# Layer-2 transposes in two row tiles of 64 tokens, with the output matmuls behind both halves

## The chip, the cores and the metric

The kernel runs on one core of one Trainium2 chip. The metric is the device time in microseconds (us) of one execution; three executions of the kernel before were timed, and their median counts. One further execution was recorded by the hardware profiler.

## What is computed

Banded attention with sinks (2 batches x 8 heads x 768 tokens, head size 64) gives 1536 token rows of 512. A first feed-forward layer (512 to 2048 to 512, squared ReLU) and a second one follow. The change is in the second layer:

```python
def _moe2_ref(x, w_in, w_out, g_ln):        # x: 1536 x 512, w_in: 512 x 1024, w_out: 1024 x 512
    h = x @ w_in
    e = np.exp(h - np.max(h, axis=-1, keepdims=True))
    sm = e / (np.sum(e, axis=-1, keepdims=True) + 1e-09)
    solu = h * sm
    mu, var = mean(solu), mean((solu - mu) ** 2)     # over the 1024 features of a token
    ln = (solu - mu) / np.sqrt(var + 1e-06) * g_ln
    return ln @ w_out
```

## The kernel before, in words

The program is written per engine, by hand: each engine runs its own list of instructions in order, and semaphores with counts tie the lists together. Nothing is scheduled by a planner. float32 matrices are split into a high and a low part (type fp32r), and each product is three matmuls: high x high, high x low, low x high.

The second layer works on 12 tiles of 128 tokens (`TILES2`). For tile i TensorE runs four pieces:

- `expand` (L1052): the tile's input, transposed, times `w_in`: 24 matmuls of 128 x 512 into two PSUM banks.
- ScalarE and VectorE then make the normed tile: VectorE the negated maximum (L849), ScalarE the exponential (L597), VectorE the product (L853), the statistics (L859 to L866), ScalarE the square root (L609), VectorE the normed rows (L874, semaphore `normed_ready`). In between VectorE also does `ln_low` of the tile before (L839) and `y_low` of a later one (L814).
- `turn_normed` (L1059): eight transposes of 128 tokens x 128 features, written as matmuls against an identity. The first four fill bank `LT_BANK`, the last four the next bank; each group of four tells `ln_turned`.
- ScalarE copies each bank to `ln_hi` (`ln_high`, L592), VectorE makes `ln_lo` from bank and `ln_hi` (`ln_low`, L839, semaphore `ln_lo_done`).
- `contract` (L1073): `ln` transposed times `w_out`, 12 matmuls for chunks 0 to 3 (half 0) and 12 for chunks 4 to 7 (half 1), into an output bank that ScalarE copies out (L587).

TensorE interleaves three tiles. In `steps(k)`, for tile i: `expand(i)`, `contract(i-2)` half 0, `turn_normed(i-1)`, `contract(i-2)` half 1. Ahead of the loop stand `expand(0)`, `expand(1)` and `turn_normed(0)`; behind it `contract(10)` half 0, `turn_normed(11)`, `contract(10)` half 1 and both halves of `contract(11)`. The first of these steps are written out, the middle ones are a hardware loop, whose waits compare with register values.

The attention part has transposes of another form: `turn` (L915) turns 64 rows x 128 columns at a time, rows 0 to 63 into one bank and rows 64 to 127 into the next, one behind the other. Trace rows name the shape of the array used: `128*128` for all rows and columns, `64*128` for half the rows, `128*64` for half the columns.

Of the kernel before, what the change touches and what calls it, by code (L numbers as in the profile page):

```python
# [8 lines left out]
P = 128  # L9
# [20 lines left out]
FC2 = D_FF2 // P  # L30
TILES2 = TOKENS // P
# [8 lines left out]
def build(nc, q_t, k_t, v, limits_in_dram, w1_in, w1_out, w2_in, w2_out, g_ln, out):  # L40
    F32, F32R, I32, U32 = mybir.dt.float32, mybir.dt.float32r, mybir.dt.int32, mybir.dt.uint32
    ALU, ACT, AX = mybir.AluOpType, mybir.ActivationFunctionType, mybir.AxisListType
# [26 lines left out]
    identity = keep.take("identity", [P, P])  # L69
# [77 lines left out]
    normed = mlp2.take("normed", [P, 2, D_FF2])  # L147
    assert mlp2.at <= BASE + 32 * KIB
    ln_hi = mlp2.take("ln_hi", [P, 2, FC2, P], F32R)
    ln_lo = mlp2.take("ln_lo", [P, 2, FC2, P], F32R)  # L150
# [14 lines left out]
    ps = nc.alloc_psum_tensor("ps", [P, 8, 512], F32)  # L165
    S_BANK, PT_BANK, X_BANK = 0, 4, 6
    H_BANK, Y_BANK = 0, 4
    LT_BANK, O_BANK = 4, 6
# [22 lines left out]
    HQ = P // 2  # L191
# [12 lines left out]
    def sem(name):  # L204
        return nc.alloc_semaphore(name)
# [67 lines left out]
    normed_ready = sem("normed_ready")  # L273
    ln_turned = sem("ln_turned")
    ln_hi_done = sem("ln_hi_done")
    ln_lo_done = sem("ln_lo_done")
# [4 lines left out]
    def wait(eng, semaphore, count):  # L281

        if isinstance(count, int) and count <= 0:
            return
        eng.wait_ge(semaphore, count)
# [14 lines left out]
    with block as block:  # L300
# [170 lines left out]
        def _(act):  # L471
# [115 lines left out]
                nc.scalar.activation(out_sb[:, u, :], ps[:, O_BANK + u, :], ACT.Copy).then_inc(out_ready, 1)  # L587

            def ln_high(i, u):
                for half in range(2):  # L590
                    act.wait_ge(ln_turned, 2 * i + half + 1)
                    nc.scalar.activation(ln_hi[:, u, 4 * half:4 * half + 4, :].rearrange("p a b -> p (a b)"), ps[:, LT_BANK + half, :], ACT.Copy).then_inc(ln_hi_done, 1)  # L592

            def tile(k, u, first, last):
                i = 2 * k + u
                act.wait_ge(ff_max_done, i + 1)
                nc.scalar.activation(expo[:, u, :], ps[:, f_bank(u):f_bank(u) + HALF2, :].rearrange("p a b -> p (a b)"),  # L597
                                     ACT.Exp, bias=ff_negmax[:, u:u + 1], accum_out=ff_sum[:, u:u + 1]).then_inc(ff_exp_done, 1)
                if first and u == 0:
                    y_out(TILES1 - 1)  # L600
                if first and u == 1:
                    act.wait_ge(y_out_dve, 2 * TILES1)
                    act.wait_ge(y_out_act, 2 * TILES1)
                if not (first and u == 0):
                    ln_high(i - 1, 1 - u)
                if not last:
                    y_high(i + 2, u)
                act.wait_ge(var_ready, i + 1)
                nc.scalar.activation(std[:, u:u + 1], var_b[:, u:u + 1], ACT.Sqrt).then_inc(std_ready, 1)  # L609
                if not first:  # L610
                    out_copy(k - 1, i - 2, u)
# [6 lines left out]
            for u in range(2):  # L618
                tile(TILES2 // 2 - 1, u, False, True)
            ln_high(TILES2 - 1, 1)  # L620
            for u in range(2):
                out_copy(TILES2 // 2 - 1, TILES2 - 2 + u, u)

        @block.vector
        def _(dve):
# [208 lines left out]


            def ln_low(i, u):
                for half in range(2):
                    dve.wait_ge(ln_hi_done, 2 * i + half + 1)
                    dve.tensor_tensor(ln_lo[:, u, 4 * half:4 * half + 4, :].rearrange("p a b -> p (a b)"), ps[:, LT_BANK + half, :],  # L839
                                      ln_hi[:, u, 4 * half:4 * half + 4, :].rearrange("p a b -> p (a b)"), ALU.subtract).then_inc(ln_lo_done, 1)  # L840

            STATS = 6

            def tile(k, u, first, last):
# [10 lines left out]
                if not (first and u == 0):  # L855
                    ln_low(i - 1, 1 - u)
# [25 lines left out]
            for u in range(2):  # L882
                tile(TILES2 // 2 - 1, u, False, True)
            ln_low(TILES2 - 1, 1)

        @block.tensor
        def _(pe):
# [158 lines left out]
            def expand(i, u):  # L1046

                pe.wait_ge(y_ready, i + 1)
                for f in range(HALF2):
                    for c in range(DC):  # L1050
                        for m, (y, w) in enumerate(((y_hi, w2_in_hi), (y_hi, w2_in_lo), (y_lo, w2_in_hi))):
                            last = mm(ps[:, f_bank(u) + f, :], y[:, u, c, :], w[:, c, 512 * f:512 * (f + 1)],  # L1052
                                      start=(c == 0 and m == 0), stop=(c == DC - 1 and m == 2))
                last.then_inc(ff_done, 1)

            def turn_normed(i, u):
                pe.wait_ge(normed_ready, i + 1)
                for f in range(FC2):
                    last = nc.tensor.transpose(ps[:, LT_BANK + f // 4, (f % 4) * P:(f % 4 + 1) * P],  # L1059
                                               normed[:, u, f * P:(f + 1) * P], identity[:, :])  # L1060
                    if f % 4 == 3:
                        last.then_inc(ln_turned, 1)

            def contract(i, u, half):

                pe.wait_ge(ln_lo_done, 2 * i + half + 1)
                if half == 0:
                    wait(pe, out_ready, i - 1)
                    if isinstance(i, int) and i < 2:
                        pe.wait_ge(y_out_dve, 2 * TILES1)  # L1070
                for f in range(FC2 // 2 * half, FC2 // 2 * (half + 1)):
                    for m, (a, w) in enumerate(((ln_hi, w2_out_hi), (ln_hi, w2_out_lo), (ln_lo, w2_out_hi))):
                        last = mm(ps[:, O_BANK + u, :], a[:, u, f, :], w[:, f, :], start=(f == 0 and m == 0), stop=(f == FC2 - 1 and m == 2))  # L1073
                if half == 1:
                    last.then_inc(out_done, 1)
# [35 lines left out]
                project(t, FC1 - 1, 1, False, True)  # L1111
            expand(1, 1)
            pe.wait_ge(y_out_act, 2 * TILES1)
            turn_normed(0, 0)

            def steps(k):
                for u in range(2):
                    i = 2 * k + u
                    expand(i, u)
                    contract(i - 2, u, 0)  # L1120
                    turn_normed(i - 1, 1 - u)
                    contract(i - 2, u, 1)

            steps(1)
            with pe.Fori(2, TILES2 // 2) as k:
                steps(k)
            contract(TILES2 - 2, 0, 0)
            turn_normed(TILES2 - 1, 1)
            contract(TILES2 - 2, 0, 1)
            for half in range(2):  # L1130
# [39 lines left out]
```

## Time and profile before

| | before |
|---|---|
| median of 3 runs | 498.95 us (497.9 to 500.12) |
| the profiled execution, its own time | 499.36 us |
| its span in the profile | 497.6 us |
| TensorE busy | 481.1 us (97%) |
| VectorE, ScalarE, GpSimd busy | 287.4, 248.0, 106.7 us |
| granted TensorE clock, whole span | 1.0 of full speed |
| second layer's stretch on TensorE | from about 350 us to the end |

The span runs from the first to the last instruction of the program; the 1.8 us between it and the execution's own time lie around it. TensorE is busy nearly throughout; a time that the second layer loses or gains on TensorE is seen one to one in the end time, as long as nothing else is late.

### The profile page before, as it was taken

What the parts mean: (1) busy time and instruction counts of PE and PEld (TensorE: products, weight loads), DVE (VectorE), ACT (ScalarE), POOL (GpSimd) and SP (SyncE); (2) the same over time, 40 slices, a digit from 0 to 9 for tenths busy, and PEclk for the clock granted to TensorE, in tenths of its full rate; (3) what the DMA queues carried; (4) which work ended last, traced back from release to release, by engine and by line L of the source; (5) the groups of instructions that cost most, each with busy time, mean ns of one, the idle gap of its engine ahead of it and who ended that gap; (6) DMA issues with size and microseconds to landing.
All of it is one profiled execution on the core that took longest, in us unless ns stands there. A gap on an engine that the chain in (4) does not pass through costs nothing.

```text
span 497.6 us, 7811 instructions
## 1 busy us (share of the span) xinstructions
PE 481.1 (97%) x2742; PEld 387.4 (78%) x2742; DVE 287.4 (58%) x678; ACT 248.0 (50%) x539; POOL 106.7 (21%) x129
## 2 busy tenths in 40 slices
PE   6889897999999999999999999999999999999997
PEld 3656575787888888888888888888888888888885
DVE  5788776368677454334435433444497666666651
ACT  3978878433443453344345334434356555545441
POOL 1876666049998000000000000000000000000000
PEclk9999999999999999999999999999999999999999
DMA  6768821170000000000000000000000000000001
GB/s 199 290 238 308 316 98 36 44 297 0 0 0 0 0 1 1 0 0 0 0 1 0 0 1 0 0 0 1 0 1 22 22 21 21 21 21 21 21 28 57
DMA packets 10138, 25.97 MB, mean 52 GB/s; under 512 B 3200, under 2 KB 5248, under 8 KB 8832
## 3 DMA queue, kind: packets, MB, share of 16 engines
q1 hardware_dynamic: 10112, 25.64, 14.1%
q8 instruction: 14, 0.23, 0.2%
q14 instruction: 12, 0.10, 0.1%
HBM read 22.48 MB, written 3.15 MB: 52 GB/s over the span
## 4 chain that ended last, share of the span: by engine, by line
PE 86%; ACT 6%; DVE 3%; DMA 3%; SPq 1%; POOL 1%; issue 1%; DVEq 0%
PE ps L1023 26%; PE ps L1038 26%; PE ps L1073 13%; PE ps L1052 13%; ACT probs L480 3%; PE ps L1059 2%; DMA k_sb<-in_k_t 2%; PE ps L951 2%; PE ps L906 1%; PE ps L915 1%; PE ps L961 1%; ACT pt_sb L488 1%; SPq L320 1%; POOL probs L402 1%; ACT x_hi L494 1%
## 5 line engine op out<-in xcount | busy, mean ns | idle before, releaser
L790 DVE CAST act_hi<-act_sq 128x512 fp32r<-128x512 f32 x48 | 26.0, 542 | 126.1 <-ACT act_sq L538 123.3
L533 ACT ACTIVATE ps<-ps 128x512 f32<-128x512 f32 x48 | 27.9, 582 | 141.4 <-PE ps L1023 141.4
L1023 PE MATMUL ps<-x_hi,w_in_hi 128*128 128x512 f32 x192 | 75.1, 391 | 0.0
L1038 PE MATMUL ps<-act_hi,w_out_hi 128*128 128x512 f32 x192 | 74.8, 390 | 0.1
L1023 PE MATMUL ps<-x_hi,w_in_lo 128*128 128x512 f32 x192 | 74.8, 389 | 0.0
L1023 PE MATMUL ps<-x_lo,w_in_hi 128*128 128x512 f32 x192 | 74.7, 389 | 0.0
L1038 PE MATMUL ps<-act_hi,w_out_lo 128*128 128x512 f32 x192 | 74.7, 389 | 0.0
L1038 PE MATMUL ps<-act_lo,w_out_hi 128*128 128x512 f32 x192 | 74.7, 389 | 0.0
L402 POOL TENSOR_TENSOR probs<-probs,row_inv 128x512 f32<-128x512 f32 (+1 forms) x48 | 45.7, 973 | 30.8 <-DVE row_inv L691 30.8
L480 ACT ACTIVATE probs<-probs,neg_max 128x272 f32<-128x272 f32 (+2 forms) x96 | 46.7, 497 | 7.1 <-DVE neg_max L678 7.0
L1023 PEld LDWEIGHTS ps<-x_hi,w_in_hi 128*128 128x128 f32 x192 | 36.0, 188 | 8.5 <-issue 1.2
L1038 PEld LDWEIGHTS ps<-act_hi,w_out_hi 128*128 128x128 f32 x192 | 36.1, 188 | 8.0 <-DVE w_out_lo L795 0.6
L1023 PEld LDWEIGHTS ps<-x_lo,w_in_hi 128*128 128x128 f32 x192 | 36.1, 188 | 7.6
L1038 PEld LDWEIGHTS ps<-act_lo,w_out_hi 128*128 128x128 f32 x192 | 36.0, 188 | 7.5
L1038 PEld LDWEIGHTS ps<-act_hi,w_out_lo 128*128 128x128 f32 x192 | 36.0, 188 | 7.4
L1023 PEld LDWEIGHTS ps<-x_hi,w_in_lo 128*128 128x128 f32 x192 | 36.0, 188 | 7.4
L1073 PE MATMUL ps<-w_out_hi,ln_hi 128*128 128x512 f32 x96 | 38.4, 400 | 0.0
L795 DVE TENSOR_TENSOR w_out_lo<-w_out_raw,w_out_hi 128x512 fp32r<-128x512 f32 x48 | 38.3, 798 | 0.0
L792 DVE TENSOR_TENSOR act_lo<-act_sq,act_hi 128x512 fp32r<-128x512 f32 x48 | 37.0, 771 | 1.7
L1073 PE MATMUL ps<-w_out_hi,ln_lo 128*128 128x512 f32 x96 | 37.5, 391 | 0.0
L1052 PE MATMUL ps<-w_in_hi,y_hi 128*128 128x512 f32 x96 | 37.4, 390 | 0.0
L1052 PE MATMUL ps<-w_in_hi,y_lo 128*128 128x512 f32 x96 | 37.4, 389 | 0.0
(97 smaller groups left out, 829.3 us busy)
## 6 DMA issues: line engine op xcount, KB each, us to landing
w_in_raw<-in_w_in SPq DMA_DIRECT2D x4, 1024.0 KB, 4.8
w_out_raw<-in_w_out SPq DMA_DIRECT2D x4, 1024.0 KB, 8.2
k_sb<-in_k_t SPq DMA_DIRECT2D x8, 408.0 KB, 5.1
q_sb<-in_q_t SPq DMA_DIRECT2D x8, 384.0 KB, 4.2
v_sb<-in_v SPq DMA_DIRECT2D x16, 192.0 KB, 3.9
out<-out_sb SPq DMA_DIRECT2D x12, 256.0 KB, 2.0
w_in_raw<-in_w_in SPq DMA_DIRECT2D x1, 2048.0 KB, 9.4
w_out_raw<-in_w_out SPq DMA_DIRECT2D x1, 2048.0 KB, 13.8
```

The source lines that it names most:

```text
L402: return pool.tensor_tensor(rows, rows, inv.to_broadcast(list(rows.shape)), ALU.mult)
L480: last = nc.scalar.activation(probs[:, b, u, cols], probs[:, b, u, cols], ACT.Exp, scale=-1.0, bias=neg_max[:, b, u, i:i + 1], accum_out=r ...
L533: nc.scalar.activation(ps[:, H_BANK + u, :], ps[:, H_BANK + u, :], ACT.Relu).then_inc(relu_done, 1)
L790: dve.tensor_copy(act_hi[:, u, :], act_sq[:, u, :]).then_inc(act_hi_done, 1)
L792: dve.tensor_tensor(act_lo[:, u, :], act_sq[:, u, :], act_hi[:, u, :], ALU.subtract).then_inc(act_lo_done, 1)
L795: dve.tensor_tensor(w1_out_lo[:, u, :], src, w1_out_hi[:, u, :], ALU.subtract).then_inc(w1_out_ready, 1)
L951: mm(ps[HEAD_DIM * u:HEAD_DIM * (u + 1), X_BANK + col // HALF, col % HALF:col % HALF + size], v_sb[:, b, u, j, :], pt_sb[:, j, width * u + ...
L1023: last = mm(ps[:, H_BANK + u, :], w[:, u, c, :], x[:, c, t * TILE1:(t + 1) * TILE1], start=(c == 0 and m == 0), stop=(c == DC - 1 and m == 2))
L1038: last = mm(ps[:, Y_BANK + c, :], w[:, u, c * P:(c + 1) * P], a[:, u, :], start=(first and m == 0), stop=(final and m == 2), skip_group_ch ...
L1052: last = mm(ps[:, f_bank(u) + f, :], y[:, u, c, :], w[:, c, 512 * f:512 * (f + 1)], start=(c == 0 and m == 0), stop=(c == DC - 1 and m == 2))
L1059: last = nc.tensor.transpose(ps[:, LT_BANK + f // 4, (f % 4) * P:(f % 4 + 1) * P], normed[:, u, f * P:(f + 1) * P], identity[:, :])
L1073: last = mm(ps[:, O_BANK + u, :], a[:, u, f, :], w[:, f, :], start=(f == 0 and m == 0), stop=(f == FC2 - 1 and m == 2))
```

## The change

The eight transposes of 128 x 128 become sixteen of 64 tokens x 128 features: for every chunk first tokens 0 to 63 (rows 0 to 63 of the array) into bank `LT_BANK`, then tokens 64 to 127 into the next bank. A bank now holds one half of the tokens of all eight chunks, and its semaphore is told at the last chunk. `ln_high` and `ln_low` read one bank each as before, and write 64 of every 128 columns. `contract` half 0 needs all tokens, so it waits for both parts of `ln_lo`; the wait in half 1 falls away. The wait for `normed_ready` moves out of `turn_normed` to the matmuls of chunk 3 in `contract` (three matmuls ahead of the transposes), and for tile 0 ahead of the first call.

```diff
             def ln_high(i, u):
-                for half in range(2):
-                    act.wait_ge(ln_turned, 2 * i + half + 1)
-                    nc.scalar.activation(ln_hi[:, u, 4 * half:4 * half + 4, :].rearrange("p a b -> p (a b)"), ps[:, LT_BANK + half, :], ACT.Copy).then_inc(ln_hi_done, 1)
+                for h in range(2):
+                    act.wait_ge(ln_turned, 2 * i + h + 1)
+                    turned_half = ps[:, LT_BANK + h, :].rearrange("p (f q) -> p f q", q=HQ)
+                    nc.scalar.activation(ln_hi[:, u, :, HQ * h:HQ * (h + 1)], turned_half, ACT.Copy).then_inc(ln_hi_done, 1)
...
             def turn_normed(i, u):
-                pe.wait_ge(normed_ready, i + 1)
+
                 for f in range(FC2):
-                    last = nc.tensor.transpose(ps[:, LT_BANK + f // 4, (f % 4) * P:(f % 4 + 1) * P],
-                                               normed[:, u, f * P:(f + 1) * P], identity[:, :])
-                    if f % 4 == 3:
-                        last.then_inc(ln_turned, 1)
+                    for h in range(2):
+                        half = slice(HQ * h, HQ * (h + 1))
+                        last = nc.tensor.transpose(ps[:, LT_BANK + h, f * HQ:(f + 1) * HQ], normed[half, u, f * P:(f + 1) * P], identity[half, half])
+                        if f == FC2 - 1:
+                            last.then_inc(ln_turned, 1)
 
             def contract(i, u, half):
 
-                pe.wait_ge(ln_lo_done, 2 * i + half + 1)
                 if half == 0:
+                    pe.wait_ge(ln_lo_done, 2 * i + 2)
                     wait(pe, out_ready, i - 1)
                     if isinstance(i, int) and i < 2:
                         pe.wait_ge(y_out_dve, 2 * TILES1)
                 for f in range(FC2 // 2 * half, FC2 // 2 * (half + 1)):
+                    if f == FC2 // 2 - 1:
+                        if not (isinstance(i, int) and i == TILES2 - 1):
+                            pe.wait_ge(normed_ready, i + 2)
                     for m, (a, w) in enumerate(((ln_hi, w2_out_hi), (ln_hi, w2_out_lo), (ln_lo, w2_out_hi))):
...
             expand(1, 1)
             pe.wait_ge(y_out_act, 2 * TILES1)
+            pe.wait_ge(normed_ready, 1)
             turn_normed(0, 0)
```

`ln_low` on VectorE changes as `ln_high` does.

TensorE's list at the middle of a loop step, around `turn_normed` (`normed` is what is turned, `ln_hi` and `ln_lo` feed the output matmuls). Before:

```order
L1073 MATMUL ps<-w_out_hi,ln_hi 128x512
L1073 MATMUL ps<-w_out_lo,ln_hi 128x512
L1073 MATMUL ps<-w_out_hi,ln_lo 128x512
L1059 MATMUL ps<-identity,normed 128x128 [waits normed_ready]
L1059 MATMUL ps<-identity,normed 128x128 x7
L1066 REGISTER_ALU
L1073 MATMUL ps<-w_out_hi,ln_hi 128x512 [waits ln_lo_done]
```

The same place with the change:

```order
L1079 MATMUL ps<-w_out_hi,ln_hi 128x512 [waits normed_ready]
L1079 MATMUL ps<-w_out_lo,ln_hi 128x512
L1079 MATMUL ps<-w_out_hi,ln_lo 128x512
L1063 MATMUL ps<-identity,normed 128x64 x16
L1079 MATMUL ps<-w_out_hi,ln_hi 128x512
```

The wait for `normed_ready` has moved three matmuls ahead, eight transposes have become sixteen, and half 1 starts without a wait.

TensorE's list at the start of the last tile's `contract`, behind the last `contract(10)` matmul. Before, where half 1 waits once more twelve matmuls later:

```order
L1073 MATMUL ps<-w_out_hi,ln_lo 128x512
L1073 MATMUL ps<-w_out_hi,ln_hi 128x512 [waits out_ready,ln_lo_done]
L1073 MATMUL ps<-w_out_lo,ln_hi 128x512
L1073 MATMUL ps<-w_out_hi,ln_lo 128x512
...
L1073 MATMUL ps<-w_out_hi,ln_lo 128x512
L1073 MATMUL ps<-w_out_hi,ln_hi 128x512 [waits ln_lo_done]
L1073 MATMUL ps<-w_out_lo,ln_hi 128x512
```

With the change:

```order
L1079 MATMUL ps<-w_out_hi,ln_lo 128x512
L1079 MATMUL ps<-w_out_hi,ln_hi 128x512 [waits out_ready,ln_lo_done]
L1079 MATMUL ps<-w_out_lo,ln_hi 128x512
L1079 MATMUL ps<-w_out_hi,ln_lo 128x512
L1079 MATMUL ps<-w_out_hi,ln_hi 128x512
```

The one wait left stands where half 0's stood, and asks for both parts of `ln_lo`.

## Rows read from the trace of the kernel before

**Rows 1.** The page: busy time by engine, and the granted clock in 40 slices.
```profile
PE 481.1 (97%) x2742; PEld 387.4 (78%) x2742; DVE 287.4 (58%) x678; ACT 248.0 (50%) x539; POOL 106.7 (21%) x129
PEclk9999999999999999999999999999999999999999
```

**Rows 2.** Chain that ended last, second layer: start us, us, what, instructions.
```profile
423.52 5.44 PE ps L1052 x24
428.96 2.72 PE ps L1073 x12
431.69 0.87 PE ps L1059 x8
432.56 2.74 PE ps L1073 x12
```

**Rows 3.** Timeline of TensorE around one turn, 430.9 to 433.2 us.
```profile
431.07 0.39 PE L1073 MATMUL ps<-w_out_lo,ln_hi 128*128 128x512 f32 x1
431.29 0.39 PE L1073 MATMUL ps<-w_out_hi,ln_lo 128*128 128x512 f32 x1
431.53 1.03 PE L1059 MATMUL ps<-identity,normed 128*128 128x128 f32 x8
432.32 0.48 PE L1073 MATMUL ps<-w_out_hi,ln_hi 128*128 128x512 f32 x1
432.63 0.40 PE L1073 MATMUL ps<-w_out_lo,ln_hi 128*128 128x512 f32 x1
```

**Rows 4.** Timeline of TensorE, cut at 88.66, then at 88.76 us.
```profile
88.64 0.28 PE L915 MATMUL ps<-identity,probs 64*128 64x64 f32 x2
...
88.64 0.34 PE L915 MATMUL ps<-identity,probs 64*128 64x64 f32 x4
```

**Rows 5.** Timeline of TensorE at the end of attention, 88.0 to 90.9 us.
```profile
88.32 0.39 PE L1023 MATMUL ps<-x_lo,w_in_hi 128*128 128x512 f32 x1
88.64 0.59 PE L915 MATMUL ps<-identity,probs 64*128 64x64 f32 x12
89.06 0.23 PE L915 MATMUL ps<-identity,sink_probs 64*128 64x64 f32 x2
89.21 1.09 PE L951 MATMUL ps<-pt_sb,v_sb 128*64 128x128 f32 x12
90.23 0.50 PE L1023 MATMUL ps<-x_hi,w_in_hi 128*128 128x512 f32 x1
90.57 0.40 PE L1023 MATMUL ps<-x_hi,w_in_lo 128*128 128x512 f32 x1
```

**Rows 6.** Durations, in ns (min/median/max), of half transposes and half-column matmuls of the attention.
```profile
L915 PE MATMUL ps<-identity,probs x352: 216/223/275, 14.6 to 89.0; 64*128 64x64 f32 x176
...
L951 PE MATMUL ps<-pt_sb,v_sb x12: 272/298/379, 89.2 to 89.9; 128*64 128x128 f32 x8, 128*64 128x256 f32 x4
```

**Rows 7.** Timeline, 371.4 to 372.6 us: TensorE, its weight loads, VectorE.
```profile
371.65 0.39 PE L1073 MATMUL ps<-w_out_hi,ln_lo 128*128 128x512 f32 x1
371.88 0.39 PE L1073 MATMUL ps<-w_out_hi,ln_hi 128*128 128x512 f32 x1
...
372.37 0.33 PEld L1059 LDWEIGHTS ps<-identity,normed 128*128 128x128 f32 x2
...
371.51 0.81 DVE L874 TENSOR_SCALAR normed<-solu,mean_var,row_gain 128x1024 f32<-128x1024 f32 x1
```

**Rows 8.** Timeline of ScalarE and VectorE before the last turn, and of TensorE.
```profile
479.32 1.09 ACT L592 ACTIVATE ln_hi<-ps 128x512 fp32r<-128x512 f32 x2 [0.69 <-PE ps L1059]
...
479.80 0.14 DVE L854 TENSOR_SCALAR ff_den<-ff_sum 128x1 f32<-128x1 f32 x1
479.95 1.29 DVE L839 TENSOR_TENSOR ln_lo<-ps,ln_hi 128x512 fp32r<-128x512 f32 x2
483.85 0.81 DVE L874 TENSOR_SCALAR normed<-solu,mean_var,row_gain 128x1024 f32<-128x1024 f32 x1
486.29 1.29 DVE L839 TENSOR_TENSOR ln_lo<-ps,ln_hi 128x512 fp32r<-128x512 f32 x2 [1.62 <-ACT ln_hi L592]
...
484.33 0.39 PE L1073 MATMUL ps<-w_out_hi,ln_hi 128*128 128x512 f32 x1
```

**Rows 9.** The same chain: the tail, from the last turn to the end.
```profile
485.19 0.87 PE ps L1059 x8
486.06 8.22 PE ps L1073 x36
```

**Rows 10.** Timeline of ScalarE and VectorE in a tile of the loop.
```profile
432.16 1.09 ACT L592 ACTIVATE ln_hi<-ps 128x512 fp32r<-128x512 f32 x2 [0.70 <-PE ps L1059]
...
437.01 0.81 DVE L874 TENSOR_SCALAR normed<-solu,mean_var,row_gain 128x1024 f32<-128x1024 f32 x1
```

More of the change, by code:

```diff
@@ L836, in ln_low @@
             def ln_low(i, u):
[L837 to L840, printed above, removed]
+                for h in range(2):
+                    dve.wait_ge(ln_hi_done, 2 * i + h + 1)
+                    queries = slice(HQ * h, HQ * (h + 1))
+                    turned_half = ps[:, LT_BANK + h, :].rearrange("p (f q) -> p f q", q=HQ)
+                    dve.tensor_tensor(ln_lo[:, u, :, queries], turned_half, ln_hi[:, u, :, queries], ALU.subtract).then_inc(ln_lo_done, 1)
             STATS = 6
@@ L1056, in turn_normed @@
             def turn_normed(i, u):
-                pe.wait_ge(normed_ready, i + 1)
                 for f in range(FC2):
-                    last = nc.tensor.transpose(ps[:, LT_BANK + f // 4, (f % 4) * P:(f % 4 + 1) * P],
-                                               normed[:, u, f * P:(f + 1) * P], identity[:, :])
-                    if f % 4 == 3:
-                        last.then_inc(ln_turned, 1)
+                    for h in range(2):
+                        half = slice(HQ * h, HQ * (h + 1))
+                        last = nc.tensor.transpose(ps[:, LT_BANK + h, f * HQ:(f + 1) * HQ], normed[half, u, f * P:(f + 1) * P], identity[half, half])
+                        if f == FC2 - 1:
+                            last.then_inc(ln_turned, 1)
             def contract(i, u, half):
-                pe.wait_ge(ln_lo_done, 2 * i + half + 1)
                 if half == 0:
+                    pe.wait_ge(ln_lo_done, 2 * i + 2)
                     wait(pe, out_ready, i - 1)
```

## The prediction, before the run

> **What bounds the kernel now.** I read the page first: TensorE is busy 97% of the span at the full granted clock, every other engine 58% or less [rows 1]. So the second layer is worth what it costs on TensorE, unless another engine becomes late. Next the chain that ended last: in the second layer it runs through TensorE alone, in a pattern that repeats every 11.78 us: 24 expanding matmuls, 12 output matmuls, 8 transposes in 0.87 us, 12 output matmuls [rows 2]. There are 12 such turns, 12 x 0.87 = 10.4 us in all, and this is what the change touches. Then the timeline around one turn, read by starts, because ends overlap: from the last full matmul's start at 431.29 to the second full one's start behind the turn at 432.63, 1.34 us go by [rows 3]. That is the measure I compare. In it, the first transpose follows the last matmul by 0.24, the eight take 0.109 each, and the first full matmul behind them holds the next back for 0.31 where 0.227 is usual.
>
> **Part 1: sixteen half transposes for eight whole ones.** The attention has exactly the new form (64*128 array, 64 rows, identity of 64), and once it stands directly behind full 128*128 matmuls, so every step has a row [rows 4 to 6].
>
> - Entry. The last full matmul starts at 88.32, the first pair of halves at 88.64 [rows 5]: 0.32. Before it was 0.24. The array has to run empty before it changes shape; no weights are loaded ahead.
> - The pairs. Two halves start together: a matmul of 0.27 and its partner span 0.28 [rows 4]. A second pair ends 0.34 - 0.28 = 0.06 later; as its matmuls take 0.223 where the first two took 0.27, it starts 0.11 behind the first. From there to the sixth pair the end moves from 0.34 to 0.59 [rows 4, 5], four steps of 0.0625. Eight pairs: 0.11 + 6 x 0.0625 = 0.485 from the first start to the last. Before, 7 x 0.109 = 0.76.
> - Exit. From the last pair at 89.06 to the next shape at 89.21: 0.15 [rows 5]. Before it was 0.03 (last transpose at 432.29, matmul at 432.32 [rows 3]; 432.29 is 431.53 + 1.03 less the 0.27 that one takes).
> - The first full matmul behind an empty array: 90.23 to 90.57, 0.34 [rows 5], against 0.31.
>
> The sum is 0.32 + 0.485 + 0.15 + 0.34 = 1.295 against 1.34: **a turn gains 0.04 us**, 12 turns 0.5 us. The transposes proper get 0.27 shorter, and the two changes of shape take back 0.23. The switch from 64*128 straight back to 128*128 is in no row; I take the one to 128*64, and bound it by 0.03 (as free as today) and by 0.31 (behind the half-column matmuls of 128*64, which end at 89.21 + 1.09 = 90.30 and take 0.379 each, a full one starts at 90.23, 0.31 behind the last start [rows 5, 6]). It should be nearest to the row of its own kind, the half transpose, behind which 23 changes of shape in the attention lie at 0.15 to 0.19, so I stay at 0.15. With the low bound a turn gains 0.16, with the high one it loses 0.12.
>
> A page of the Trainium skill, "TensorEngine Tiling (Array Packing)", section Key Properties, says that a change of tiling mode drains the array. Another, "TensorE: Matmul & The Clock Gate", section Single matmul latency, gives a lone bf16 matmul of N columns (398+N)/2.4 ns, 0.38 us for 512 and 0.19 for 64. An estimate with these as the two drains would make a turn dearer by 0.06 and 0.04 than my sum, so that it loses 0.06 in place of gaining 0.04, and the kernel would take some 1.0 us more; the trace's 0.32 and 0.15 are shorter, and I use them.
>
> **Part 2: the wait for the normed tile, three matmuls earlier.** In the loop it costs nothing: the tile is ready at 437.82 [rows 10] and the turn that uses it comes at about 443.3, one 11.78 us period behind 431.53. Twice there is no such slack.
>
> - Turn of tile 1. VectorE ends the tile at 372.32, and TensorE's weight load for the transposes starts at 372.37, just in time [rows 7]. The wait now sits on the matmul that started at 371.88. It would start at 372.37, 0.49 late, with nothing loaded ahead (0.34 in place of 0.227, so 0.11 more): 0.61 us later than before. The 0.04 that turn 0 gained is swallowed.
> - Turn of tile 11. The tile is ready at 484.66 [rows 8]; the matmul that now waits started at 484.33 [rows 8]. With 0.05 for the signal that is 0.38. A bank is now complete only at the end of the turn: ScalarE started 0.63 behind the first transpose (432.16 against 431.53 [rows 10, 3]); now it is 0.08 (later entry) + 0.485 + 0.22 + 0.04, some 0.2 later. `ln_lo`, which started at 479.95 right behind 479.80 + 0.14 [rows 8], is then held up by 0.15, and the statistics and the normed tile behind it on VectorE too. So 0.53, and 0.11 for the empty array: 0.64. Turn 10's gain is swallowed as well.
>
> Turns 1 to 9 and 11 keep their gain, 10 x 0.04 = 0.4. **Net: 0.61 + 0.64 - 0.4 = +0.85 us.**
>
> **Part 3: output matmuls behind both halves.** In the loop `ln_lo` is done one whole `expand` (5.44) before its use; nothing. Only the end is close: the last `ln_lo` ended at 487.58 [rows 8], and the last tile's matmuls start at 486.06 + 2.74 = 488.80 [rows 9, 2]. The later bank costs 0.25 of that 1.2 us. Nothing again, and without that cover it would come at most to those 0.25 us. `ln_hi` and `ln_lo` are written in pieces of 64 elements; both are off the path, with 5 us of slack in the loop, so this costs nothing unless they double.
>
> **The sum** against the profiled execution's own 499.36 us: 500.2. That execution stands 0.4 above the median of 498.95, so for the median of runs I forecast **499.8 us**.
>
> **The rivals.**
>
> 1. *The earlier wait is harmless* (the halves and loads flow around it, or it holds nothing back). Then only the 12 x 0.04 stay: 498.5. Against it: both tiles are ready later than the matmul that now asks for them [rows 7, 8]. Chance 0.12.
> 2. *Row tiling doubles the rate and the changes of shape are hidden.* A turn falls from 0.87 to 0.435. The two late waits stay, and swallow turns 0 and 10: 0.61 + 0.64 - 10 x 0.435 = -3.1, so 495.8, faster. Against it: pairs come every 0.0625, but the 0.32 and 0.15 around them are in the trace [rows 5]. The Trainium skill, "TensorEngine Tiling (Array Packing)", section Theoretical Speedup, states up to 2x for a dimension of 64 or less; the attention's rows bear this out inside a block (0.0625 for a pair against 0.109), not at its edges. Chance 0.07.
> 3. *The halves do not overlap here*, slower: each takes its own slot of 0.0625, 14 or so in place of 7. A block of 16 then takes 0.11 + 14 x 0.0625 = 0.99 in place of 0.485, 0.5 a turn; 10 turns lose 0.46 each: 0.61 + 0.64 + 4.6 = 5.9, so 504.8. It decides from about 0.02 us between the halves of a pair on. For it: the banks and operands are new. Against it: 352 rows of the attention at 0.22 [rows 6], in pairs [rows 4]. Chance 0.05.
> 4. *The way back to the full shape is dearer*, up to the 0.31 bound: 0.16 a turn more, +1.6, so 501.4, or with more than that slower. Chance 0.08, half of it above the bound of "same".
>
> That the change does not do what it says can hardly be: the list of instructions shows sixteen transposes and the moved wait.
>
> **How the numbers follow.** My own case has 0.68. A measurement of this kernel can tell about 0.5%, 2.5 us, from no change: below 496.45 is faster, above 501.45 slower. Same: 0.68 + 0.12 + 0.04 = 0.84; slower: 0.05 + 0.04 = 0.09; faster: 0.07. The range takes in rival 1 and the bounds of the exit (a gain of 0.16 a turn would give 498.6, a loss of 0.12 some 501.4) and a little for the scatter of a median: 498.0 to 501.6.
>
> **What would show it right or wrong.** In the new trace: halves starting in pairs 0.06 apart; from the last full matmul's start to the second full one's behind the turn about 1.30 us; the period still about 11.74; TensorE idle some 0.5 us at two places only, ahead of the fourth chunk in the first and the last `contract` before a turn, with VectorE's normed tile named as releaser; the last `ln_lo` done about 0.9 us before it is wanted. A distance of 0.95 or less would mean the shape changes are hidden; 1.45 or more would be rival 3 or 4; no idle time at the two places, rival 1.

## The result, and the profile after

| | before | changed |
|---|---|---|
| median of 12 runs | 498.75 us (497.71 to 500.12) | 499.91 us (499.03 to 500.82) |
| ratio to before | | 1.0026, 95% interval 1.0017 to 1.0036 |
| span of the profiled execution | 497.6 us | 499.0 us |
| TensorE, first `expand` matmul to the last matmul's start | 144.00 us | 144.97 us |
| from the last full matmul to the second full one behind a turn (typical) | 1.337 us | 1.299 us |

The change costs 1.2 us (1.16 between the medians; the interval says 0.8 to 1.8). The forecast was 0.85 us over a median of 498.95, so 499.8. The fourth line takes the second layer alone: the stretch ahead of it varies by some 1.5 us between profiled executions, whatever the kernel (the first `expand` started between 348.8 and 350.4 us), while one kernel that was profiled twice (e1 and e9 below) had second layers of 143.574 and 143.573 us. It grew by 0.97 us, which lies inside the interval for the whole kernel. The ratios of the experiments below leave out two slow executions, one of e1 (541.4 us) and one of the kernel before beside it (1230.16 us), which the medians keep.

The page of the changed kernel, busy time by engine, and the granted clock, against [rows 1]:

```profile
PE 482.6 (97%) x2838; PEld 384.6 (77%) x2838; DVE 285.3 (57%) x678; ACT 248.1 (50%) x539; POOL 107.4 (22%) x129
PEclk9999999999999999999999999999999999999999
```

There are 96 matmuls more (8 more for each of 12 turns). The granted clock and the counts of the other engines are as before; VectorE's busy time is 2.1 us less and that of the weight loads 2.8 us less, neither of them the bound. The timeline of TensorE around one turn of the loop, against [rows 3] (start us, us, engine, line, operation, count):

```profile
431.99 0.39 PE L1079 MATMUL ps<-w_out_lo,ln_hi 128*128 128x512 f32 x1
432.22 0.39 PE L1079 MATMUL ps<-w_out_hi,ln_lo 128*128 128x512 f32 x1
432.54 0.71 PE L1063 MATMUL ps<-identity,normed 64*128 64x64 f32 x16
433.18 0.50 PE L1079 MATMUL ps<-w_out_hi,ln_hi 128*128 128x512 f32 x1
433.52 0.40 PE L1079 MATMUL ps<-w_out_lo,ln_hi 128*128 128x512 f32 x1
```

"Full" matmuls are those of 128x512 on the whole array, "halves" the half transposes. Read it by starts: 0.32 to the first half, then 0.49 to the last one (0.71 less the 0.22 that one takes), 0.15 to the first full matmul, 0.34 to the second: 1.30 us. The same view cut at 432.6 and at 432.7 us shows the pairs, as [rows 4] do:

```profile
432.54 0.28 PE L1063 MATMUL ps<-identity,normed 64*128 64x64 f32 x2
...
432.54 0.34 PE L1063 MATMUL ps<-identity,normed 64*128 64x64 f32 x4
```

Two halves end 0.28 us after the start, four 0.34: the partners of a pair start together, within 4 ns, and a second pair costs 0.06. In the 12 turns the distance from the last full matmul to the second one behind the turn is 1.299 to 1.304; before it was 1.332 to 1.339.

What pays for this saving, and more, are two idle times. TensorE ahead of the turns of tile 1 and tile 11, against [rows 7, 8] (in brackets the idle time and its releaser):

```profile
372.08 0.39 PE L1079 MATMUL ps<-w_out_hi,ln_lo 128*128 128x512 f32 x1
372.85 0.50 PE L1079 MATMUL ps<-w_out_hi,ln_hi 128*128 128x512 f32 x1 [0.38 <-DVE normed L876]
373.19 0.39 PE L1079 MATMUL ps<-w_out_lo,ln_hi 128*128 128x512 f32 x1
...
484.87 0.39 PE L1079 MATMUL ps<-w_out_hi,ln_lo 128*128 128x512 f32 x1
485.71 0.50 PE L1079 MATMUL ps<-w_out_hi,ln_hi 128*128 128x512 f32 x1 [0.45 <-DVE normed L876]
```

From start to start 0.77 us and 0.84 us go by where 0.227 is usual: 0.54 and 0.61 us lost. The matmul behind is followed at 0.34 in place of 0.227, so 0.11 more each. No other gap in the second layer's matmuls is longer than a turn's own. VectorE's end of the normed tile fits: 371.99 + 0.81 = 372.80, and 0.05 later the matmul starts; for tile 11 it is 484.84 + 0.81 = 485.65, and 0.06.

```profile
371.99 0.81 DVE L876 TENSOR_SCALAR normed<-solu,mean_var,row_gain 128x1024 f32<-128x1024 f32 x1
...
484.84 0.81 DVE L876 TENSOR_SCALAR normed<-solu,mean_var,row_gain 128x1024 f32<-128x1024 f32 x1
```

The sum for the second layer: 0.54 + 0.61 + 2 x 0.11 - 12 x 0.038 = 0.91 us, of 0.97 measured. The rest, some 0.05, is spread over the 559 ordinary steps from one full matmul to the next, which take 227.35 ns in the mean and took 227.26 before; why is not shown.

The later bank can be seen on VectorE before the turn of tile 11, against [rows 8]:

```profile
480.59 0.14 DVE L856 TENSOR_SCALAR ff_den<-ff_sum 128x1 f32<-128x1 f32 x1
480.95 1.29 DVE L842 TENSOR_TENSOR ln_lo<-ps,ln_hi 128x512 fp32r<-128x512 f32 x2 [0.21 <-ACT ln_hi L593]
```

Before, `ln_lo` started 0.15 behind `ff_den` and did not wait for ScalarE; now it starts 0.36 behind and does: 0.21 later, and all that stands behind it on VectorE with it.

The joint wait ahead of the last tile's output matmuls is met in time. The last `ln_lo` ended at 487.98 + 1.29 = 489.27, and the first matmul that needs it started at 490.12, at the usual distance behind the one ahead of it:

```profile
487.98 1.29 DVE L842 TENSOR_TENSOR ln_lo<-ps,ln_hi 128x512 fp32r<-128x512 f32 x2 [2.33 <-ACT ln_hi L593]
```

### The profile page after: what moved, and what is told of

Its sections match the earlier page's. It is cut to its first block, busy times and chain, and to the rows that moved or that the text cites. A ratio compares the mean times of both kernels' runs of the same rounds, so it can differ in the third digit from the quotient of the medians.

```text
span 499.0 us, 7995 instructions
## 1 busy us (share of the span) xinstructions
PE 482.6 (97%) x2838; PEld 384.6 (77%) x2838; DVE 285.3 (57%) x678; ACT 248.1 (50%) x539; POOL 107.4 (22%) x129
## 4 chain that ended last, share of the span: by engine, by line
PE 84%; ACT 5%; DVE 4%; DMA 2%; SPq 1%; issue 1%; POOL 1%; DVEq 0%
PE ps L1025 26%; PE ps L1040 26%; PE ps L1079 12%; PE ps L1054 12%; ACT probs L480 3%; DMA k_sb<-in_k_t 2%; PE ps L908 2%; PE ps L953 2%; PE ps L1063 1%; PE ps L917 1%; PE ps L963 1%; ACT pt_sb L488 1%; SPq L320 1%; POOL probs L402 1%; ACT x_hi L494 1%
## 5 line engine op out<-in xcount | busy, mean ns | idle before, releaser
L791 DVE CAST act_hi<-act_sq 128x512 fp32r<-128x512 f32 x48 | 21.5, 448 | 128.2 <-ACT act_sq L538 125.3
L793 DVE TENSOR_TENSOR act_lo<-act_sq,act_hi 128x512 fp32r<-128x512 f32 x48 | 38.4, 799 | 1.7
L782 DVE TENSOR_TENSOR w_in_lo<-w_in_raw,w_in_hi 128x512 fp32r<-128x512 f32 x48 | 37.7, 787 | 1.7 <-ACT w_in_hi L523 1.7
L1079 PE MATMUL ps<-w_out_lo,ln_hi 128*128 128x512 f32 x96 | 37.4, 390 | 0.0
```

The costliest lines, as they stand in the source:

```text
L782: dve.tensor_tensor(w1_in_lo[:, u, :, :], src, w1_in_hi[:, u, :, :], ALU.subtract).then_inc(w1_in_ready, 1)
L791: dve.tensor_copy(act_hi[:, u, :], act_sq[:, u, :]).then_inc(act_hi_done, 1)
L793: dve.tensor_tensor(act_lo[:, u, :], act_sq[:, u, :], act_hi[:, u, :], ALU.subtract).then_inc(act_lo_done, 1)
```

## The experiments

The first question was whether the loss comes from the two late waits or from something spread over the turns. Intervals are of the ratio to runs of the kernel before on the same chip. The ratios differ a little from the quotients of the medians beside them (e2: 500.20 / 498.73 = 1.0029), and the intervals hold both. "Second layer" is the fourth line of the table above, read from each profile.

| run | ratio, 95% interval | median, us | before, us | second layer against before |
|---|---|---|---|---|
| e1_wait_at_turn | 0.9987 (0.9972 to 1.0001) | 498.39 | 498.73 | -0.42 |
| e2_wait_alone | 1.0020 (1.0004 to 1.0036) | 500.20 | 498.73 | +1.08 |
| e3_both_halves_alone | 1.0007 (0.9998 to 1.0016) | 499.22 | 498.73 | -0.03 |
| e4_wait_at_chunk_0 | 1.0176 (1.0159 to 1.0194) | 507.47 | 498.73 | +8.22 |
| e5_rows_in_turn | 1.0061 (1.0040 to 1.0082) | 502.21 | 499.15 | +3.21 |
| e6_turn_in_two_parts | 1.0075 (1.0048 to 1.0102) | 502.89 | 499.15 | +4.00 |
| e7_wait_at_chunk_2 | 1.0046 (1.0028 to 1.0063) | 501.17 | 498.78 | +2.31 |
| e8_wait_at_chunk_1 | 1.0096 (1.0077 to 1.0115) | 503.59 | 498.78 | +3.73 |
| e9_wait_at_turn_again | 0.9997 (0.9984 to 1.0010) | 498.65 | 498.78 | -0.43 |

### Row tiles without the two late waits

```diff
             def turn_normed(i, u):
+                if isinstance(i, int):
+                    pe.wait_ge(normed_ready, i + 1)
...
-                    if f == FC2 // 2 - 1:
-                        if not (isinstance(i, int) and i == TILES2 - 1):
-                            pe.wait_ge(normed_ready, i + 2)
+                    if f == FC2 // 2 - 1 and not isinstance(i, int):
+                        pe.wait_ge(normed_ready, i + 2)
...
-            pe.wait_ge(normed_ready, 1)
             turn_normed(0, 0)
```

Only the written-out steps have whole numbers for i, and these hold the turns of tiles 0, 1, 2 and 11.

> The row-tiled transposes stay; at the turns of tiles 1, 2 and 11 (and 0) the wait for the normed tile goes back to the first transpose, in the loop it stays at chunk 3, where the tile is long ready. Theory (two late waits cost 0.61 and 0.64 us, the row-tiled turns gain 0.04 each): 12 x 0.04 = 0.5 us faster than before, some 1.7 us faster than the change's 499.9. TensorE never idle ahead of those turns. Rival (the loss is spread over all turns, in the changes of array shape): no better than the change, about 1.1 us slower than before.

Measured: ratio 0.9987, second layer 0.42 us shorter than before. The timeline of TensorE at the turn of tile 11:

```profile
484.42 0.39 PE L1079 MATMUL ps<-w_out_hi,ln_lo 128*128 128x512 f32 x1
484.73 0.72 PE L1064 MATMUL ps<-identity,normed 64*128 64x64 f32 x16
485.38 0.50 PE L1079 MATMUL ps<-w_out_hi,ln_hi 128*128 128x512 f32 x1
```

The 0.32 to the first half is that of every turn; nothing waits. With the waits where they were, the change's loss of 0.97 turns into a gain of 0.42. The same kernel was run once more, with 11 executions beside the 12 of the first time:

> The first of these experiments once more, for a narrower interval: row-tiled transposes, the wait of tiles 0, 1, 2 and 11 at their first transpose. Theory: 0.4 to 0.5 us faster than before, ratio 0.999. Rival (the gain seen in the trace is given back elsewhere): ratio 1.000 or more.

The second layer gained the same 0.43 us, but the ratio is 0.9997 with 1 inside the interval. So the gain is plain in the trace, and the time of the whole kernel does not resolve it. Against the change the version is clearly better (its intervals end at 1.0001 and 1.0010, that of the change begins at 1.0017); against the kernel before it is no better that one could measure.

### The wait alone

In the kernel before, with its whole transposes, the waits stand as in the change (same lines as in the diff of the change), and nothing else is touched.

> The kernel before with its whole 128x128 transposes, and only the wait for the normed tile moved to chunk 3 of the output matmuls. Theory: tile 1 costs 0.49 + 0.11 = 0.60 us, tile 11 costs 0.38 + 0.11 = 0.49 us (its normed tile is not held up by a later bank): 1.1 us slower than before. Rival (the wait hurts only together with the row tiles): equal to before within 0.2 us.

Measured 1.0020, second layer +1.08 us. TensorE idles at the same two places:

```profile
371.45 0.39 PE L1076 MATMUL ps<-w_out_hi,ln_lo 128*128 128x512 f32 x1
372.17 0.50 PE L1076 MATMUL ps<-w_out_hi,ln_hi 128*128 128x512 f32 x1 [0.33 <-DVE normed L874]
...
484.49 0.39 PE L1076 MATMUL ps<-w_out_hi,ln_lo 128*128 128x512 f32 x1
485.10 0.50 PE L1076 MATMUL ps<-w_out_hi,ln_hi 128*128 128x512 f32 x1 [0.22 <-DVE normed L874]
```

Lost are 713 - 227 = 486 ns and 606 - 227 = 379 ns, read from the starts to the nanosecond, and 0.11 twice: 1.08, all that was measured. The forecast said 0.49 and 0.38. In the change the second is 0.61 where it is 0.38 here; that 0.23 is the later bank, 0.21 by VectorE's rows above, and the time that turn 10 had gained.

### Both halves alone

```diff
-                pe.wait_ge(ln_lo_done, 2 * i + half + 1)
                 if half == 0:
+                    pe.wait_ge(ln_lo_done, 2 * i + 2)
```

> The kernel before, and only the output matmuls' wait changed: both parts of ln_lo ahead of half 0, none ahead of half 1. Theory: 0.0 us against before, within 0.2 us, since the second part is ready a whole expand early in the loop and 1.2 us early at the end. Rival (the joint wait costs in the last tile, where it has least cover): 0.3 to 0.7 us slower, with TensorE idle behind L1073 ahead of the last tile's output matmuls.

The second layer is 0.03 us shorter than before, and the last tile's first output matmul follows the one ahead at 0.227 us as everywhere: no wait. The ratio of 1.0007 has 1 in its interval. The joint wait is free, here and in the change.

### The place of the wait, moved step by step

The changed kernel with `if f == 0`, `if f == 2` or `if f == 1` in place of `if f == FC2 // 2 - 1`. First chunk 0, nine matmuls further ahead:

> The changed kernel with the wait for the normed tile nine matmuls further ahead, at chunk 0 of the output matmuls. Theory (the wait's place is the cost, in the first and the last tile alone): each of the two late waits grows by 9 x 0.227 = 2.04 us, so 4.1 us slower than the change and 4.9 us slower than before; in the loop nothing, as the tile is ready 2.7 us ahead of chunk 0. Rival (the wait is not what costs): equal to the change, about 1.1 us slower than before. Rival (it costs in every tile): 10 x 0.5 us or more beyond that.

It took 8.2 us in the second layer, not the 4.9 of the theory and not the 1 of the first rival. The steps in the loop were as short as in the change (11.75 and 11.77 us from turn to turn), so it did not cost in every tile either. The missing 3.3 us lie at and, most of them, behind the two waits. TensorE around the first:

```profile
368.95 0.39 PE L1054 MATMUL ps<-w_in_hi,y_lo 128*128 128x512 f32 x1
371.85 0.58 PE L1079 MATMUL ps<-w_out_hi,ln_hi 128*128 128x512 f32 x1 [2.51 <-DVE normed L876]
372.23 0.63 PE L1079 MATMUL ps<-w_out_lo,ln_hi 128*128 128x512 f32 x1
372.65 0.63 PE L1079 MATMUL ps<-w_out_hi,ln_lo 128*128 128x512 f32 x1
373.08 0.63 PE L1079 MATMUL ps<-w_out_hi,ln_hi 128*128 128x512 f32 x1
```

Starts are 0.427 us apart in place of 0.227. The view of stretches gives the clock granted in each (stretch, then its length, busy time by engine, PEclk):

```profile
366.00:368.90 2.90, 2.90 (x14) 2.42 (x13) 2.90 (x6) 2.42 (x4) 0.00 (x0) 1.00 0.00 0
371.80:375.00 3.20, 3.15 (x8) 2.52 (x9) 1.93 (x2) 1.21 (x2) 0.00 (x0) 0.54 0.02 5
488.40:491.20 2.80, 2.80 (x7) 2.22 (x8) 0.00 (x0) 0.00 (x0) 0.00 (x0) 0.50 0.27 99
```

Behind each idle time (2.51 and 2.58 us) the clock was at its lower level of 1.2 GHz, half of 2.4, for some 3 us: seven or eight matmuls at 0.2 us more. By their starts this cost 1.6 us at the first place and 1.4 at the second, 3.0 together. The idle times themselves grew by 2.13 us each over those of the change, not by the 2.04 of nine matmuls, and the theory had started from a change of 0.85 and not 0.97; that is the rest of the 3.3. Two smaller steps tell the two effects apart:

> The changed kernel with the wait for the normed tile three matmuls further ahead, at chunk 2. The kernel with the wait at chunk 0 lost 8.7 us in place of 4.9: its two waits left TensorE idle for 2.5 us or more each, and the matmuls behind them ran at half the clock for a while. Theory (the place costs 0.227 us per matmul of either tile, as long as the clock holds): 2 x 0.68 us on top of the change, 2.4 us slower than before, granted clock 1.0 throughout. Rival (any longer idle time already costs clock): 1 to 4 us more than that.

> The changed kernel with the wait at chunk 1, six matmuls further ahead. Theory: 2 x 1.36 us on top of the change, 3.7 us slower than before if the clock holds through idle times of about 1.9 us; each of the two waits behind which it falls adds some 1.7 us (eight matmuls at 0.427 in place of 0.227), so 5.4 us with one and 7.1 us with both.

Second layer +2.31 and +3.73 us, against forecasts of 2.4 and 3.7. Here are the first waits of the two kernels, chunk 2 and then chunk 1:

```profile
371.91 0.50 PE L1079 MATMUL ps<-w_out_hi,ln_hi 128*128 128x512 f32 x1 [1.03 <-DVE normed L876]
```

```profile
372.65 0.50 PE L1079 MATMUL ps<-w_out_hi,ln_hi 128*128 128x512 f32 x1 [1.74 <-DVE normed L876]
```

The second waits are of 1.11 and 1.80 us. In both kernels the clock stayed at 1.00 in the stretches behind. So the series is 0.97, 2.31, 3.73 in even steps of 1.3 to 1.4 (2 x 3 x 0.227 = 1.36), and then 8.22, a step of 4.5, where the clock falls.

### The halves in another order

On the kernel of the first experiment:

```diff
-                for f in range(FC2):
-                    for h in range(2):
+                for h in range(2):
+                    for f in range(FC2):
```

> As the kernel with the waits put back at the turns of tiles 1 and 11, but the sixteen half transposes in another order: all eight of tokens 0 to 63, then all eight of tokens 64 to 127, so that neighbours use the same rows of the array. Theory (only neighbours on different rows go together): every half takes a slot of 0.0625 us of its own, 14 slots in place of 6, about 0.5 us more per turn, 6 us in all: 5.5 us slower than before. Rival (the 0.0625 is the pace at which pairs of instructions are supplied, whatever the rows): no difference to the alternating order, 0.5 us faster than before.

Second layer +3.21 us, 3.63 more than with the alternating order: 0.30 us a turn, between the theory's 0.5 and the rival's 0. The timeline of one turn:

```profile
443.86 0.39 PE L1079 MATMUL ps<-w_out_hi,ln_lo 128*128 128x512 f32 x1
444.18 1.01 PE L1064 MATMUL ps<-identity,normed 64*128 64x64 f32 x16
445.12 0.50 PE L1079 MATMUL ps<-w_out_hi,ln_hi 128*128 128x512 f32 x1
```

From the first half's start to the last it is 0.79 us (1.01 less 0.22) in place of 0.49. Start by start, the halves come singly, 0.06 apart, then for the middle of the block in twos, and singly again. The likely reading is that the second row group's halves begin beside the last ones of the first group: the half that starts 0.302 us behind the first one takes 0.273, as only the first half of each group does elsewhere (0.272, the others 0.22), and with it the starts fall into two series of eight. The records do not name the rows, so that is inferred. What is shown is that the order decides, and that the supply of instructions does not: the same sixteen come faster alternating. Neighbours of this order share the output bank as well as the rows, and no run separates the two. The 0.32 ahead and the 0.15 behind are unchanged.

### The changes of shape doubled

On the kernel of the first experiment, the transposes of chunks 4 to 7 of tiles 1 to 11 stand three matmuls later, inside half 1:

```diff
-                    turn_normed(i - 1, 1 - u)
-                    contract(i - 2, u, 1)
+                    turn_normed(i - 1, 1 - u, part=0)
+                    contract(i - 2, u, 1, turns=(i - 1, 1 - u))
...
                 for f in range(FC2 // 2 * half, FC2 // 2 * (half + 1)):
+                    if turns and f == FC2 // 2 + 1:
+                        turn_normed(*turns, part=1)
```

> As the kernel with the waits put back at the turns of tiles 1 and 11, but the turns of tiles 1 to 11 split: chunks 0 to 3 at the old place, chunks 4 to 7 three matmuls later, inside half 1. It doubles the number of changes of array shape and nothing else. Theory (a change of shape empties the array, at fixed cost): a part takes 0.32 + 0.11 + 2 x 0.0625 + 0.15 + 0.34 = 1.045 us from full matmul to second full matmul; two parts 2.09 less the 1.295 of a whole turn and the two slots of 0.227 they take in: 0.34 us per turn, 11 turns 3.7 us: 3.2 us slower than before. Rival (the gaps at the edges are the supply of instructions or the waits, and not the shape): under 0.1 us per turn, about 0.5 us faster than before to 0.6 slower.

```profile
432.38 0.39 PE L1081 MATMUL ps<-w_out_hi,ln_lo 128*128 128x512 f32 x1
432.70 0.46 PE L1064 MATMUL ps<-identity,normed 64*128 64x64 f32 x8
433.09 0.50 PE L1081 MATMUL ps<-w_out_hi,ln_hi 128*128 128x512 f32 x1
433.43 0.39 PE L1081 MATMUL ps<-w_out_lo,ln_hi 128*128 128x512 f32 x1
433.66 0.40 PE L1081 MATMUL ps<-w_out_hi,ln_lo 128*128 128x512 f32 x1
433.99 0.46 PE L1064 MATMUL ps<-identity,normed 64*128 64x64 f32 x8
```

Each part shows the full price at its edges: 0.32 in, 0.15 out, 0.34 to the second full matmul. From full matmul to second full one a part takes 1.05 us, as expected. Two parts make a turn 0.35 us dearer, 11 turns 3.8, and the second layer is 4.43 longer than that of the first experiment. Another 0.43 is a new wait: both banks are now complete only at the later part, and the turn of tile 11 starts 0.43 us late behind VectorE's normed tile. The last 0.2 is spread over the ordinary steps between full matmuls (227.7 ns in the mean, 227.3 in the first experiment). The forecast of 3.2 us over the kernel before had neither of these two; 4.00 was measured.

## Why the prediction was right

The sum was right in sign and in its parts, and a little low in size. That 499.8 lies within 0.1 us of the measured median is in part luck: the median of three it started from was 0.2 us above that of twelve, and the cost of 0.85 was 0.1 below the second layer's 0.97 and 0.3 below the 1.16 of the medians. Step by step:

- *Entry, pairs, exit, first full matmul.* 0.32 + 0.485 + 0.15 + 0.34 = 1.295 was forecast, 1.299 measured. That the rows of the attention would hold for another place, another pair of banks and a switch straight back to the full shape was a choice, and the exit was the one term without a row. It came at 0.153, at the value of the half transposes' own rows, and not at either bound. The upper bound of 0.31 was of another kind: it stood behind matmuls of 0.379, and goes with their length (see the last section). The estimate by the Trainium skill ("TensorE: Matmul & The Clock Gate", section Single matmul latency), by which a turn would lose 0.06, was 0.10 us a turn too dear. The rule of the Trainium skill that a change of tiling mode drains TensorE ("TensorEngine Tiling (Array Packing)", section Key Properties) agrees with the trace as far as this can show it: 0.32 in place of 0.23 on the way in, 0.15 in place of 0.03 on the way out, and e6 shows the price paid once more for each further pair of changes.
- *Gain per turn.* 0.04 forecast, 0.038 measured (1.337 less 1.299).
- *The waits.* For tile 1, 0.49, plus 0.04 as the turn ahead had gained time, against 0.54. For tile 11, 0.53 and the same 0.04, against 0.61. The small miss is the later bank: 0.15 was worked out, 0.21 measured. 0.11 behind each was right. (0.49 + 0.11 is 0.60; the prediction wrote 0.61.)
- *Both halves.* Nothing forecast, nothing found, in e3 and in the change. The cover was read 0.1 too large: in the kernel before, the last tile's matmuls start at 488.66, 1.08 us behind `ln_lo`, and not at 488.80. The change left 0.85 of it, where about 0.9 was named.
- *Rival 1*, the harmless wait, is excluded by e2 (1.0020, lower end of the interval 1.0004) and by the idle times with their releaser. *Rival 2*, hidden changes of shape, falls with the distance of 1.30 and with e6. *Rival 3*, halves that do not overlap, falls with the pairs. Its size, 0.5 us a turn, may have been too high: with neighbours on the same rows the turn grew by only 0.30. *Rival 4*, a dearer way back, falls with the 0.153.

What the forecasts did not see lay beside the change itself: that of e4 held a stall at a flat price for each matmul of distance. In the second layer that is so up to idle times of 1.80 us, and no longer at 2.51.

## What to carry to other kernels

Cost a smaller array shape by what stands at its edges, not by its pace inside: here the block itself fell from 0.76 to 0.49 us and the two changes of shape took back all but 0.04. By these figures it pays more in longer blocks, or next to others of the same shape; no run here tried that. Before moving a wait ahead on the busiest engine, look at the first and the last step, where the pipeline has no slack, and not at the loop, where it has 5 us. And put the halves of a row-tiled group in alternating order.

## What was unexpected

- The clock's price for idle time: in the second layer TensorE kept the full clock through idle times of up to 1.80 us; behind 2.51 and 2.58 us the matmuls came 0.427 us apart at 1.2 GHz for some 3 us. One step of three matmuls in a wait's place then cost 4.5 us in place of 1.4. The length of one idle time does not settle it alone: near the start of the program, in e6, TensorE idled for 2.11 us and worked from 6.49 to 7.87 us with the clock at 1.00, and from 7.9 us on, idle again, it was granted 0.50.
- Half transposes on the same rows, one behind the other, are not fully serial: 0.79 us for sixteen, where fifteen single slots of 0.06 would be 0.9.
- A matmul of the next array shape started 0.07 us ahead of the recorded end of the one before wherever nothing else held it up: 0.32 behind a full matmul recorded with 0.39, 0.15 behind a half transpose with 0.22, and in the attention 0.20 behind a half-column matmul with 0.27 and 0.31 behind one with 0.379. So in this kernel the recorded length of the last matmul gives the distance at a change of shape behind it.
